# Linear attention and two gated products on one core: a product with w_k inside the last chunk pair, scans ahead of the first weighing, another cut of the last tile

## What is computed

```python
batch, n_heads, seq, head_dim = (2, 8, 768, 64)
# per block: intra-block scores with a decay mask, and a running state
intra = np.einsum('bhic,bhjc->bhij', qb, kb) * Dmask[None]
intra = np.einsum('bhij,bhjd->bhid', intra, vb)
inter = np.einsum('bhid,bhde->bhie', qb * lam_pow[None], kv_state)
out[:, :, sl] = intra + inter
kv_state = lam_block * kv_state + np.einsum('bhsd,bhse->bhde', kb_dec, vb)
...
xk = mu_k * x + (1.0 - mu_k) * x_prev
xr = mu_r * x + (1.0 - mu_r) * x_prev
k = np.maximum(xk @ w_k, 0.0)
v = k * k @ w_v
r = 1.0 / (1.0 + np.exp(-(xr @ w_r)))
x = r * v
...
gate_pre += conv_w[k][None, None, :] * xp[:, k:k + S, :]   # 5 taps
gate = 1.0 / (1.0 + np.exp(-gate_pre))
val = x @ w_val
return (gate * val @ w_out).astype(np.float32)
```

## Time and profile before

| | us |
|---|---|
| median of 3 runs | 278.47 (278.42 to 278.76) |
| the profiled execution | 278.52 |
| its span in the trace | 276.5 |
| PE busy | 269.3 (97%) |
| DVE / ACT / POOL busy | 167.4 / 125.3 / 48.5 |

### The profile page before, as it was taken

How to read it: one execution, slowest core, us unless ns; L and a number is a source line. 1 busy time by engine, 2 the same in 40 slices (tenths; PEclk the granted TensorE clock), 3 DMA queues, 4 the chain that set the end, 5 groups by cost and what they waited for, 6 DMA issues and landing times.

```text
span 276.5 us, 4258 instructions
## 1 busy us (share of the span) xinstructions
PE 269.3 (97%) x1740; PEld 225.8 (82%) x1740; DVE 167.4 (61%) x248; ACT 125.3 (45%) x223; POOL 48.5 (18%) x35
## 2 busy tenths in 40 slices
PE   8799988999999999999999999999999999999996
PEld 8689977888888888888888888888888888888885
DVE  4956981899979113455886545337978599425000
ACT  2137758769477213457821143749217305412121
POOL 1667757916900000000000000000000000000000
PEclk9999999999999999999999999999999999999999
DMA  6999996000000000000000000350000000310323
GB/s 234 417 400 413 407 407 245 0 0 2 0 0 0 2 0 0 0 0 2 0 0 0 4 1 0 116 190 0 0 0 2 0 0 0 116 38 0 114 78 114
DMA packets 7506, 22.83 MB, mean 83 GB/s; under 512 B 960, under 2 KB 1216, under 8 KB 7488
## 3 DMA queue, kind: packets, MB, share of 16 engines
q1 hardware_dynamic: 7488, 22.57, 21.2%
HBM read 19.42 MB, written 3.15 MB: 82 GB/s over the span
## 4 chain that ended last, share of the span: by engine, by line
PE 94%; DVE 2%; issue 1%; ACT 0%
PE ps L697 28%; PE ps L695 28%; PE ps L696 28%; PE ps L763 4%; PE ps L711 3%; PE ps L750 2%; PE ps L728 1%; DVE qdec L598 1%; DVE pT L505 0%; DVE state L522 0%; ACT out_sb L412 0%; DVE state L519 0%; DVE om L600 0%
## 5 line engine op out<-in xcount | busy, mean ns | idle before, releaser
L695 PE MATMUL ps<-xk_h,wk_h 128*128 128x512 f32 x96 | 37.5, 390 | 0.0
L697 PE MATMUL ps<-xk_h,wk_l 128*128 128x512 f32 x96 | 37.4, 389 | 0.0
L696 PE MATMUL ps<-xk_l,wk_h 128*128 128x512 f32 x96 | 37.4, 389 | 0.0
L695 PE MATMUL ps<-kk_h,wv_h 128*128 128x512 f32 x96 | 37.3, 389 | 0.0
L696 PE MATMUL ps<-kk_l,wv_h 128*128 128x512 f32 x96 | 37.3, 389 | 0.0
L697 PE MATMUL ps<-kk_h,wv_l 128*128 128x512 f32 x96 | 37.3, 389 | 0.0
L568 DVE SCALAR_TENSOR_TENSOR gate<-x,prm,gate 128x512 f32<-128x512 f32 x48 | 32.6, 745 | 0.0
L544 DVE SCALAR_TENSOR_TENSOR kk_f<-ps,ring 128x512 f32<-128x512 f32 x24 | 16.5, 688 | 23.8 <-ACT ring L365 23.8
L382 ACT ACTIVATE gate<-x,prm 128x512 f32<-128x512 f32 x12 | 8.6, 724 | 38.8 <-DVE x L554 38.8
L365 ACT ACTIVATE ring<-ps 128x512 f32<-128x512 f32 x24 | 14.3, 597 | 26.0 <-PE ps L697 26.0
L549 DVE TENSOR_TENSOR kk_l<-kk_f,kk_h 128x512 fp32r<-128x512 f32 x24 | 21.2, 883 | 1.8 <-ACT kk_h L369 1.8
(11 more groups left out here) (72 smaller groups left out, 499.7 us busy)
## 6 DMA issues: line engine op xcount, KB each, us to landing
qk<-in_qk SPq DMA_DIRECT2D x12, 512.0 KB, 11.0
kv<-in_kv SPq DMA_DIRECT2D x10, 512.0 KB, 12.0
out<-out_sb SPq DMA_DIRECT2D x11, 256.0 KB, 2.0
wk_raw<-in_w_k SPq DMA_DIRECT2D x4, 512.0 KB, 13.4
wv_raw<-in_w_v SPq DMA_DIRECT2D x4, 512.0 KB, 11.7
wr_raw<-in_w_r SPq DMA_DIRECT2D x2, 512.0 KB, 15.1
w_raw<-in_w_val SPq DMA_DIRECT2D x2, 512.0 KB, 4.5
w_raw<-in_w_out SPq DMA_DIRECT2D x2, 512.0 KB, 6.9
```

Of the source, the lines that this page charges most:

```text
L695: nc.tensor.matmul(to, left(0), right(0), start=(i == 0), stop=False)
L696: nc.tensor.matmul(to, left(0), right(1), start=False, stop=False)
L697: done = nc.tensor.matmul(to, left(1), right(0), start=False, stop=(i == last))
```

## The change

Five things are altered.

- `hidden(0, 0)` stands between `inter(11)` and `attend(10)`. Its weights come sooner: ACT takes the high part of `wk` piece 0 ahead of `fade(9)`, and POOL, no longer DVE, takes its low part, right behind `decay_q(11)`.
- The scans of `qdec` stand ahead of `weigh(0)`; on POOL `decay_q(1)` stands ahead of `decay_k(1)`; on PE `update(1)` stands behind `attend(1)`.
- SP loads `qk` of chunk 2 ahead of `kv` of chunk 1, and `qk` of chunk 3 ahead of `kv` of chunks 2 and 3.
- The dummies are 12 products of 84 columns where they were 8 of 128.
- The last output chunk is cut at column 384: parts of 384 and of 128 columns.

```diff
-WARM = 8
+WARM, WARM_COLS = 12, 84
+CUTS = (0, 384, DM)
...
             load_kv(0)
+            load_qk(2)
             load_kv(1)
-            for p in range(1, NP - 1):
+            load_qk(3)
+            load_kv(2)
+            load_kv(3)
+            for p in range(2, NP - 1):
...
             decay_k(0)
-            decay_k(1)
             pool.wait_ge(qdec_ok, PAIRS)
             decay_q(1)
+            decay_k(1)
...
-            for i in range(1, 4):
+            for i in range(4):
                 low(wk, wk_raw, i, wk_hi, wk_lo)
...
             evacuate_x(3)
+            high(wk, wk_raw, 0, wk_here, wk_hi)
             fade(9)
...
-            for i in range(3):
+            for i in range(1, 3):
                 high(wk, wk_raw, i, wk_here, wk_hi)
...
-            weigh(0)
             dve.wait_ge(zero_ok, 1)
...
+            weigh(0)
             nc.vector.tensor_scalar(om[:, :], prm[:, MU:MU + 2 * KT], -1.0, 1.0, ALU.mult, ALU.add).then_inc(om_ok, 1)
...
-                if p == 5:
-                    low(wk, wk_raw, 0, wk_hi, wk_lo_first)
...
-                if t == 0 and n == 0:
-                    pe.wait_ge(wk_lo_first, 1)
-                elif t == 0 and n % 2 == 0:
-                    pe.wait_ge(wk_lo, n // 2)
+                if t == 0 and n % 2 == 0:
+                    pe.wait_ge(wk_lo, n // 2 + 1)
...
-                    halves = [(bank, 0, DM // 2), ((bank + 1) % 8, DM // 2, DM)]
+                    halves = [((bank + i) % 8, CUTS[i], CUTS[i + 1]) for i in range(2)]
...
             scores(2)
-            update(1)
             inter(1)
             attend(1)
+            update(1)
...
                 inter(2 * p + 1)
+                if p + 1 == NP:
+                    hidden(0, 0)
                 attend(2 * p)
...
-                for n in range(FT):
+                for n in range(1 if t == 0 else 0, FT):
```

More of the change, by code:

```diff
@@ L147, in build @@
             sem(z) for z in "wk_hi wk_lo wr_hi wr_lo wv_hi wv_lo w2_hi w2_lo".split()]
-        wk_lo_first = sem("wk_lo_first")
         (xk_part, xk_full, xk_hi, xk_lo, xr_part, xr_full, xr_hi, xr_lo) = [
@@ L260, in _ @@
                     for half in range(2):
-                        cols = slice(half * DM // 2, (half + 1) * DM // 2)
+                        cols = slice(CUTS[half], CUTS[half + 1])
                         sp.wait_ge(out_ready, n + 1 + half)
@@ L409, in evacuate @@
                     for half in range(2):
-                        cols = slice(half * DM // 2, (half + 1) * DM // 2)
+                        cols = slice(CUTS[half], CUTS[half + 1])
                         act.wait_ge(proj_done, n + 1 + half)
                         nc.scalar.copy(out_sb[t][:, c, cols],
-                                       ps[:, (bank_of("proj", t, c) + half) % 8, 0:DM // 2]).then_inc(out_ready, 1)
+                                       ps[:, (bank_of("proj", t, c) + half) % 8, 0:CUTS[half + 1] - CUTS[half]]).then_inc(out_ready, 1)
             act.wait_ge(warm_ok, 1)
@@ L852, in _ @@
             for _ in range(WARM):
-                nc.tensor.matmul(ps[:, 7, 0:P], warm[:, :], warm[:, :], start=True, stop=True)
+                nc.tensor.matmul(ps[:, 7, 0:WARM_COLS], warm[:, :], warm[:, 0:WARM_COLS], start=True, stop=True)
             scores(0)
```

## The result

| | before | changed |
|---|---|---|
| median of 6 runs each | 278.50 us (278.42 to 278.76) | 280.88 us (280.71 to 283.0) |
| ratio to before | | 1.0086, 95% interval 1.0063 to 1.011 |
| the profiled execution, its span | 278.52, 276.5 | 281.3, 279.1 |

The account below looks back on a forecast made before the run. PE was taken as the bound, busy 269.3 us of a 276.5 us span. 278.52, plus 2.2 for the later value(0, 0), plus 0.3 at the end, gave 281.0 us; range 279.2 to 282.6.

Parts of the forecast that it names:

- The last pair: Chunks 10 and 11: POOL's wk_l delays DVE's second L535 to 42.55, so inter(11) starts at 43.05, the product at 43.65.
- the sum: The main step-by-step timeline on the profiled execution: value(0, 0) at 80.0 instead of 77.81, total 281.0 us.
- The size of PE's wait: At inter(11), PE waits some 2.5 us for DVE's state, with the head's gain inside that wait.
- That depends on the load, so it stays: In the last pair, kdec of chunk 10 starts with its load at 35.30; both qd end at 39.06.
- The chain: From attend(11) through xr_f to the last kk_l: 31.86 us, 0.81 to spare; now kk_l at 79.85, holding value(0, 0).
- What the product gives: hidden(0, 0), 2.73 us, ahead of the last attends: their 0.80 gap goes, leaving 2.15 to 2.3 us for both.
- GpSimd's part: In the last pair, POOL's wk_l from 39.6 to 42.0 holds DVE's second L535 until 42.55 instead of 40.21.
- The head: Program start up to scores(4): earlier scans, new orders and loads, more dummies; some 0.8 us won, zero cost on the path.
- Won, and not kept: Some 0.8 us gained at the head, scores(4) then held by its load until 16.6, the gain lost inside inter(11)'s wait.
- my two ends: The 12 dummies at the head: no change if columns count, or 1.9 us later if each costs 0.47.
- The end: Last output chunk: 12 narrow matmuls at 0.115 make PE 0.58 later, smaller copy and store return 0.3: plus 0.3.
- The clock: Rival: at the 2.5 us wait the clock drops to 1.2 GHz, hidden(0, 0) takes twice its 2.73, 283.7 us; chance 0.05.

Follow-up runs that it names:

- e6: Kernel before with hidden(0, 0) moved, its low part on GpSimd, and GpSimd's four low parts of w_v left out: 278.59 us, ratio 0.9994.
- e12: Kernel before with hidden(0, 0) moved, its low part on VectorE, and GpSimd's four low parts of w_v left out: 278.01 us, ratio 0.9968.
- e11: The changed kernel as it is, run again in one session with e9: 280.87 us, ratio 1.0072.
- e7: Kernel before with only the head's scans, decays, update(1) and loads of the change; dummies, product and cut as before: 278.55 us, ratio 0.999.
- e1: Changed kernel with hidden(0, 0) back behind attend(11), its low part still on POOL: 279.39 us, ratio 1.0023.
- e5: Kernel before with hidden(0, 0) moved and its high part early, but its low part left on VectorE: 279.70 us, ratio 1.0031.
- e2: Kernel before with only hidden(0, 0) moved, its high part early and its low part on GpSimd: 280.94 us, ratio 1.0076.
- e9: Changed kernel with w_k's first low part back on VectorE behind the last state: 280.51 us, ratio 1.0062.
- e8: Changed kernel with 8 dummies of 128 columns again instead of 12 of 84: 280.96 us, ratio 1.0082.
- e3: Kernel before with only the dummies changed, to 12 of 84 columns: 279.28 us, ratio 1.0034.
- e10: e7 with 4 dummies of 256 columns instead of 8 of 128: 278.63 us, ratio 0.9995.

## Why the prediction was right, point by point

- *The last pair.* Right, almost to the row. The second `xk_l` done at 42.69 (forecast 42.55), `inter(11)` at 43.16 (43.05), the product at 43.76 (43.65), ACT's copy at 48.75 (48.7), GpSimd's last `wr_l` done at 58.36 (58.4), `value(0, 0)` at 79.97 (80.0). PE alone would have been at 43.76 plus 34.9 (e6, e12), 78.66; the sum had 78.65.
- *How close it came* is in part luck. From `kdec` to `inter(11)` the sum has 7.75 and the profiles 7.3; `kdec` was 0.52 late, and the two nearly cancel. The product took 2.97 (forecast 2.73), the two `attend` behind it 1.90 (2.15 to 2.3). In e11, the same program, `value(0, 0)` starts at 80.40.
- *The size of PE's wait* was wrong. I had some 2.5 us at the last `inter`; it was 0.57, and 1.58 in e11. The step that failed is that PE keeps the head's gain up to there. In the changed kernel it never has it: `scores(4)` starts at 17.50, 0.07 earlier than before, and the gap that ends at 31.32 makes PE 1.1 us later than before at `inter(8)` (31.85 for 30.77). With the old dummies (e7) it has the gain, and gives it back in such a gap. The sum was not hurt, since it went by VectorE's times.
- *"That depends on the load, so it stays"*: the load does not stay. `kdec` started between 35.03 and 36.34 over the profiles. The forecast took 35.30; the changed kernel's profile had 35.82, and `kdec` was 0.20 shorter there (1.08 for 1.28).
- *The chain.* Right. It costs 1.3 us over PE's own pace (36.2 against 34.9); the sum had 1.35. The four L529 took 6.98 (forecast 6.9). e6 and e12 show that it is this chain.
- *What the product gives.* The gap at the last `attend` went, as the sum assumed. It also goes in e1, where no product stands ahead but PE has waited 1.55 us for the state: PE must only come late enough. From the end of `inter(11)` to `value(0, 0)` was 35.86 before; without the chain it is 34.9. So the 2.16 us are 1.81 for the later start, minus 0.96, plus 1.31.
- *The split between GpSimd's part and the chain* is less firm than the sum. By e5 against e2 the first is 1.2 us, by e9 against e11 0.4, by the distances 0 to 1.0.
- *The head.* "Won, and not kept" is right (e7, e8), but not by the path I gave. `scores(4)` is held by its load only with the old dummies (16.51 in e7, 16.36 in e8); in the changed kernel it starts at 17.50, with no wait. The dummies cost 1.6 us (till 6.47 for 4.83), and the slow pace held until 10.2 in this profile (the first 32 `scores` took 3.79); in e11, the same program, it ended sooner (2.98). Of my two ends the upper, 1.9, was the near one. Alone they cost 0.9 us (e3, interval 0.3 to 1.6); in the changed kernel the last state covers that (e8).
- *The end.* 0.3 measured, 0.3 forecast, of 0.53 up to the last copy (forecast 0.58) less 0.2 for copy and store (0.3); a product of 128 columns every 0.112 us (nine steps from 275.54 to 276.55), for 0.115. The weight load gave the right size; that it is the cause no run shows by itself. By the Trainium skill's rule for the load ("TensorE: Matmul & The Clock Gate", section "LDWEIGHTS (loading the stationary operand)") the sum would have been 0.35: the trace agrees with it too.
- *The clock* did not fall: the changed kernel's page grants it in full in every slice, through the waits of 0.57 and 1.13 us. A wait of 2.5 us did not come up.

## What to carry to other kernels

Before a product is moved ahead of a stage to fill a gap, follow what leaves that stage to its next meeting with the moved engine: here the product was worth 0.9 us to PE and cost the chain through VectorE 1.3 us beyond its slack. A helper instruction given to an idle engine is not free if it shares VectorE's turns: ask which short instructions it will stand against, and who waits behind them. And a gain at the head counts only up to the next thing that does not move with it, a load or the fetch of PE's next instructions.

The traces point to a version that was not run: e5 with ACT's three casts of `w_k` and `w_r` ahead of the last copy of `x`, since ACT idles 4.18 us there and the casts (2.9 us) now stand in the chain. If their loads are there in time, the chain would lose its 1.13 us of wait, and the kernel would come near e12. That is argued, not shown.

## What the runs showed of the hardware that was not expected

- A gap released by "issue" sits at a fixed count of PE's instructions and moves with the number of dummies (behind 22, 14 or 6 matmuls for 8, 16 or 24 dummy records), and the next one comes 124 matmuls, with their 124 weight loads, later. The first gap of e3, behind 32 `scores`, is the one exception. What PE waits for there the traces let one infer: a DMA queue of the kind "instruction" brings 14 packets of 16 KB over the span (its row below: packets, MB, share), and PE's 1740 matmuls (1748 in the changed kernel) hold 124 fourteen times. In the 14 profiles the other 25 gaps all end 2.39 to 2.62 us behind the start of such a packet (36.04 and 38.60 in the changed kernel, 36.75 and 39.16 in e10). Where a packet starts early enough there is no gap: in `scores(9)` of the changed kernel it started at 28.93, 0.20 behind `scores(8)`, and the gap of 0.77 followed; in e11, the same program, it started at 28.04, 1.26 ahead, and there was none. Why it starts earlier in some executions is open.
- These gaps have 0.2 to 0.9 us of listed idle time, in the stretch in which the loads run at 395 to 416 GB/s (the other row below, 7.0 us a slice). The Trainium skill, "Runtime: NRT & Kernel Launch", section "Instruction fetch mechanics", has the crossing from one block of code to the next mostly hidden; here it is not, in this stretch. That the loads are the cause was not tried, and the packets' own times do not bear it out: they take 1.0 to 1.1 us each from 13 to 44 us, and 0.9 to 1.5 later, when little else is moved. The rival, not tried either, is that the matmuls are short here: 124 of them take some 7 us in attention and 28 us in the layers, where packets come 28 us apart and PE waits for none.

```profile
q8 instruction: 14, 0.23, 0.3%
GB/s 253 416 395 412 407 404 211 1 0 2 0 0 0 0 2 0 0 0 2 0 0 0 4 1 0 79 224 0 0 0 2 0 0 0 115 38 0 113 77 113
```

- Fp32 dummies of 84 columns are no cheaper than those of 128, and above that the columns count: 0.225 us a pass for 84 columns, 0.236 for 128, and 0.47 for 256 (8 passes in 3.78), so that 4 of 256 do the work of 8 of 128 in the same time.
- Kernels with the same head start their fifth `scores` anywhere from 16.85 to 17.67 us (e5, e2): a difference of under 1 us between two profiles of this kernel needs a distance between two points of the same trace, not two absolute times.
